# Down products with the upper halves one block ahead, later waits for expert vectors and padding, and logits placed among wide products

## The reference

```python
# 1. retention, per head, gamma = 1 - 2**(-5 - h)
state = gamma * state + k[t] v[t]^T
y[t] = scale * q[t] @ state
# 2. MLP, d_ff = 2048
h = x @ w_in
x = (maximum(h, 0) + alpha * minimum(h, 0)) @ w_out
# 3. top-1 mixture of 8 experts, d_ff = 1024
logits = (x / |x|) @ (emb / |emb|).T / tau
e = argmax(logits);  gate = softmax(logits)[e]
out = gate * (maximum(x @ w1[e], 0) @ w2[e])
```

## Time and profile before

| | us |
|---|---|
| median of 3 runs | 992.33 |
| lowest and highest | 988.33, 994.5 |
| the profiled execution | 989.66 |
| its span, first to last instruction | 987.8 |
| PE busy, PEld busy | 960.6 (97%), 794.4 (80%) |
| DVE, ACT, POOL busy | 579.2, 256.5, 241.3 |
| mean granted clock of TensorE | 0.993 of full |

### The profile page before, as it was taken

One profiled execution on the slowest core, in us unless ns is written; L12 is line 12 of the kernel. 1 busy time (PEld: TensorE's weight loads), 2 busy tenths in 40 slices (PEclk: granted clock), 3 DMA queues, 4 the chain that ended last, 5 costly groups with the idle time before them and its releaser, 6 DMA issues.

```text
span 987.8 us, 16560 instructions
## 1 busy us (share of the span) xinstructions
PE 960.6 (97%) x5448; PEld 794.4 (80%) x5449; DVE 579.2 (59%) x1079; ACT 256.5 (26%) x405; POOL 241.3 (24%) x192
## 2 busy tenths in 40 slices
PE   7999999999999999999999999999999999999994
PEld 6788778888887888878887888877888888888883
DVE  4655579637973698459864878664332742524541
ACT  4222121112111211122111212332333533423541
POOL 3443114241433133413441224210000110000000
PEclk9999999999999999999999999999999999999998
DMA  7431393023001400140011203446331361423310
GB/s 283 157 139 55 116 370 114 1 86 129 0 0 73 140 0 0 43 149 1 1 44 54 107 35 134 130 136 249 128 128 43 150 262 43 175 75 121 125 44 31
DMA packets 27122, 100.48 MB, mean 102 GB/s; under 512 B 4383, under 2 KB 4767, under 8 KB 22448
## 3 DMA queue, kind: packets, MB, share of 16 engines
q1 hardware_dynamic: 19136, 80.64, 22.8%
q0 software_dynamic: 4336, 12.61, 3.3%
q10 hardware_dynamic: 3600, 6.58, 2.4%
HBM read 87.19 MB, written 24.20 MB: 113 GB/s over the span
## 4 chain that ended last, share of the span: by engine, by line
PE 88%; DVE 4%; DMA 2%; SPq 1%; ACT 1%; issue 1%; POOL 1%; ACTq 0%; DVEq 0%; POOLq 0%
PE bank L684 25%; PE bank L675 25%; PE bank L759 14%; PE bank L785 14%; PE bank L571 2%; PE bank L770 2%; PE bank L617 2%; PE bank L587 1%; PE bank L660 1%; PE bank L604 1%; DMA en_all<-en_rows 1%; DVE scratch L898 1%; DVE scratch L903 1%; DMA en_all<-in_qk 1%; DVE activations_split L909 1%
## 5 line engine op out<-in xcount | busy, mean ns | idle before, releaser
L684 PE MATMUL bank<-weights_split,activations_split 128*128 128x512 f32 x1152 | 278.7, 391 | 4.9 <-DVE activations_split L909 4.7
L675 PE MATMUL bank<-activations_split,weights_split 128*128 128x512 f32 x1152 | 277.5, 391 | 0.4 <-issue 0.4
L684 PEld LDWEIGHTS bank<-weights_split,activations_split 128*128 128x128 f32 x1152 | 215.2, 188 | 54.6 <-DVE activations_split L909 7.8
L675 PEld LDWEIGHTS bank<-activations_split,weights_split 128*128 128x128 f32 x1152 | 215.1, 188 | 45.8 <-issue 1.5
L1478 POOL TENSOR_TENSOR activations_split<-scratch,activations_split 128x512 fp32r<-128x512 f32 x84 | 118.0, 1405 | 332.5 <-ACT activations_split L1266 325.1
L1266 ACT CAST activations_split<-scratch 128x512 fp32r<-128x512 f32 x96 | 59.8, 622 | 418.1 <-DVE scratch L903 418.1
L785 PE MATMUL bank<-weights_split,activations_split 128*128 (+1 forms) x648 | 154.9, 394 | 3.0 <-DVE activations_split L1130 2.2
L759 PE MATMUL bank<-weights_split,activations_split 128*128 (+1 forms) x648 | 156.8, 398 | 0.5 <-DVE activations_split L1107 0.5
L785 PEld LDWEIGHTS bank<-weights_split,activations_split 128*128 128x128 f32 x648 | 119.6, 188 | 27.5 <-issue 3.6
L759 PEld LDWEIGHTS bank<-weights_split,activations_split 128*128 128x128 f32 x648 | 121.3, 191 | 24.8 <-issue 0.7
L960 DVE SCALAR_TENSOR_TENSOR attention<-rows,en_all 128x512 f32<-128x512 f32 x140 | 135.0, 1006 | 0.0
(11 more groups left out here) (183 smaller groups left out, 678.4 us busy)
## 6 DMA issues: line engine op xcount, KB each, us to landing
attention<-in_w_exp SPq DMA_DIRECT2D x24, 1024.0 KB, 4.8
attention<-in_kv SPq DMA_DIRECT2D x43, 256.0 KB, 3.8
expert_rows<-in_pad_rows SPq DMA_DIRECT2D x8, 1028.0 KB, 18.3
en_all<-in_w_exp SPq DMA_DIRECT2D x8, 1024.0 KB, 7.1
rows<-in_w_mlp SPq DMA_DIRECT2D x14, 512.0 KB, 3.4
rows<-expert_rows ACTq DMA_DIRECT2D x25, 257.0 KB, 2.7
attention<-in_qk SPq DMA_DIRECT2D x12, 512.0 KB, 4.9
scratch<-in_qk SPq DMA_DIRECT2D x10, 512.0 KB, 3.7
```

The lines of the kernel that those rows point to most:

```text
L675: last = mm(H_ps[f % 2][:, :], win(a, kc, f), x[:, kc, :], start=(k == 0), stop=(k == 3 * KC - 1))
L684: last = mm(bank[j][:, :], x[f % 2][:, j * P:(j + 1) * P], wout(a, f), start=(f == 0 and n == 0), stop=(f == FB - 1 and n == 2))
```

## The change

In `down`, the twelve products of a block keep their operands but take another order: the two products with the upper half of the activations for group i come first, and the product with the lower half follows one group later. The block waits for `s_gh` at its start and for `s_gl` ahead of its fifth product. The order of the groups' last products is then 5th, 8th, 11th and 12th. `expert_down` does the same within each half of four feature blocks. In the first expert tile, the logits of group j are made behind the three products of feature block j of the second up half. DVE's wait for the expert vectors moves into `dots`, behind block 0's activations. ACT's wait for the padding moves behind `relu_half(2)` and `x_hi_part(3, 3)`, and the rows of tile 5 are loaded by SP instead of ACT.

```diff
--- before.py
+++ after.py
@@ -539,6 +539,7 @@
             sp.wait_ge(s_pad0, due(s_pad0, 16))
             sp.wait_ge(s_pads, due(s_pads, 16 * E))
             load_rows(sp, 1, 0)
+            load_rows(sp, 1, 1)
             with sp.Fori(2, E) as p:
                 e = sp.value_load(tab[0:1, bass.ds(T_PERM + p, 1)], min_val=0, max_val=E - 1)
                 for m in range(NCH):
@@ -677,13 +678,22 @@
                         k += 1
                 last.then_inc(s_h, 1)
 
+            def high_first(n):
+
+                order = []
+                for i in range(n):
+                    order += [(i, 0, "hi"), (i, 1, "hi")] + ([(i - 1, 0, "lo")] if i else [])
+                return order + [(n - 1, 0, "lo")]
+
             def down(c, f):
-                pe.wait_ge(s_gl, due(s_gl, FB * c + f + 1))
-                for j in range(B):
-                    for n, (a, x) in enumerate(((0, g_hi), (1, g_hi), (0, g_lo))):
-                        last = mm(bank[j][:, :], x[f % 2][:, j * P:(j + 1) * P], wout(a, f),
-                                  start=(f == 0 and n == 0), stop=(f == FB - 1 and n == 2))
-                    if f == FB - 1 and j < B - 1:
+                pe.wait_ge(s_gh, due(s_gh, FB * c + f + 1))
+                for n, (j, a, part_) in enumerate(high_first(B)):
+                    if n == 4:
+                        pe.wait_ge(s_gl, due(s_gl, FB * c + f + 1))
+                    x = g_hi if part_ == "hi" else g_lo
+                    last = mm(bank[j][:, :], x[f % 2][:, j * P:(j + 1) * P], wout(a, f),
+                              start=(f == 0 and a == 0 and part_ == "hi"), stop=(f == FB - 1 and part_ == "lo"))
+                    if f == FB - 1 and part_ == "lo" and j < B - 1:
                         last.then_inc(s_x2, 1)
                 last.then_inc(s_X, 1)
 
@@ -746,7 +756,7 @@
             def expert_of(t):
                 return pe.value_load(tab[0:1, bass.ds(T_EXP + t, 1)], min_val=0, max_val=E - 1)
 
-            def up(t, tt, half, e):
+            def up(t, tt, half, e, between=None):
                 slot = e % 2
                 if half == 0:
                     pe.wait_ge(s_el, due(s_el, t + 1))
@@ -760,7 +770,11 @@
                                   W[:, bass.ds(slot * HALF + w1_at(kc, a) + half * 512, 512)],
                                   start=(k == 0), stop=(k == 3 * KC - 1))
                         k += 1
+                    if between is not None and kc < KC - 1:
+                        between(kc)
                 last.then_inc(s_M1, 1)
+                if between is not None:
+                    between(KC - 1)
 
             def h_transpose(t):
                 for half in range(HF):
@@ -776,12 +790,14 @@
                 pe.wait_ge(s_lo[1], due(s_lo[1], HC * e))
                 pe.wait_ge(s_yd, due(s_yd, t))
                 k = 0
-                for fc in range(FC):
-                    if fc % 4 == 0:
-                        pe.wait_ge(s_hl, due(s_hl, 2 * t + fc // 4 + 1))
-                    if fc == FC // 2 and between is not None:
+                for half in range(HF):
+                    if half and between is not None:
                         between()
-                    for a, x in ((0, eh_hi), (1, eh_hi), (0, eh_lo)):
+                    pe.wait_ge(s_hh, due(s_hh, 2 * t + half + 1))
+                    for n, (i, a, part_) in enumerate(high_first(4)):
+                        if n == 4:
+                            pe.wait_ge(s_hl, due(s_hl, 2 * t + half + 1))
+                        x, fc = eh_hi if part_ == "hi" else eh_lo, 4 * half + i
                         last = mm(EY_ps[:, :], x[tt % 2][:, fc * P:(fc + 1) * P],
                                   W[:, bass.ds(slot * HALF + w2_at(fc, a), DM)],
                                   start=(k == 0), stop=(k == 3 * FC - 1))
@@ -803,9 +819,7 @@
             up(0, 0, 0, 0)
             for j in range(B):
                 last_transpose(j)
-            for j in range(B):
-                last_logits(j)
-            up(0, 0, 1, 0)
+            up(0, 0, 1, 0, between=last_logits)
             router_rank(NC - 1)
             mm(CNT_ps, ones, seen[:, :, B], start=True, stop=True).then_inc(s_cnt, 1)
             up(1, 1, 0, 0)
@@ -954,6 +968,8 @@
                 if first == 0:
                     dve.wait_ge(s_xeV, due(s_xeV, 2 * c + 2))
                     dve.wait_ge(s_xeA, due(s_xeA, 2 * c + 2))
+                    dve.wait_ge(s_en_all, due(s_en_all, 16))
+                    dve.wait_ge(s_en_last, due(s_en_last, 1))
                 for n in range(first, first + count):
                     j, e = n // E, n % E
                     dve.wait_ge(s_lg, due(s_lg, B * E * c + max(n - 1, 0)))
@@ -1089,8 +1105,6 @@
             ve.reciprocal(tau_sb[:, :], TAU_ps).then_inc(s_ent, 1)
 
             attention(1)
-            dve.wait_ge(s_en_all, due(s_en_all, 16))
-            dve.wait_ge(s_en_last, due(s_en_last, 1))
             def chunk(c):
                 mlp(c - 1, router_c=c - 2)
                 rows_out(c - 1)
@@ -1396,14 +1410,15 @@
             x_hi_part(2, 2)
             y_part(1, 0, 1)
             act.wait_ge(s_tab, due(s_tab, 1))
-            act.wait_ge(s_pads, due(s_pads, 16 * E))
             w1_part(next_expert(2), 1)
             relu_half(2)
             x_hi_part(3, 3)
+            act.wait_ge(s_pads, due(s_pads, 16 * E))
 
             def tile(i, tt, e):
                 t = 4 * i + tt
-                load_rows(act, i, tt + 3)
+                if not (isinstance(t, int) and t == 2):
+                    load_rows(act, i, tt + 3)
                 h_hi_part(t, tt)
                 e_next = next_expert(t + 1)
                 w1_part(e_next, t)
```

## The result

| | before | after |
|---|---|---|
| median | 991.83 us (4 runs, 988.33 to 994.5) | 980.59 us (4 runs, 979.11 to 981.26) |
| profiled execution | 989.66 | 980.66 |
| its span | 987.8 | 978.8 |

The ratio is 0.9896, with a 95% interval from 0.9871 to 0.992: faster by 1.0%. The forecast was 981.7 us, 1.1 us too high. The profiled executions are 9.0 us apart, where the sum said 10.6. So the total agrees better than its parts, and the parts are what is worth reading.

The account below looks back on a forecast made before the run. TensorE (PE), 88% of the chain, was taken as the bound, so time lay in its gaps and slow clock. Terms 2.3 + 5.5 + 0.75 - 0.4 + 1.0 + 0.75 + 0.7 = 10.6 us; 992.3 - 10.6 = 981.7 us, range 976 to 988.5.

Parts of the forecast that it names:

- The wait for the vectors: The 2.39 us gap before mlp(1)'s down products closes once DVE waits for the expert vectors later: 2.3 us gained.
- the ten gaps: Gaps before down products of each chunk's first and last hidden blocks close with upper halves first: 5.5 us gained.
- the POOL gaps: Two last-chunk gaps, 0.67 and 0.34 us, ended by POOL's low half, close: 0.75 us gained.
- kind (a): Gaps of 0.65 us before down products of a chunk's first and last hidden blocks, ended by DVE's low halves.
- The yardstick: A PEld gap is not lost whole, since the first load after it waits for nothing: 0.13 us off each gap.
- the second rival: In down blocks the fifth product still waits, its release costing 0.3 us: gain 8.1 us, 984.2 us; chance 10%.
- the third rival: Bank changes inside down blocks cost time: 480 more changes, up to 62 us, 1044 us; chance 3%.
- The end of a chunk: Banks complete later, so ACT's copies delay the start of attention in chunks 2 to 4: 0.4 us lost.
- The logits: Last chunk's logits among wide products: 1.0 us gained if the clock holds, despite a new 1.9 us rank-product stall.
- The first rival: The clock falls again around the last logits and rank products: about 3 us lost, 984.7 us; chance 22%.
- The padding: In the expert stage, ACT's later padding wait lets tile 2's relu finish before tile 3's transposes: 0.75 us gained.
- The last tile: Last expert tile's down products start on the upper half, shortening the 2.40 us gap: 0.7 us gained.

Follow-up runs that it names:

- vectors_alone: The kernel before with only DVE's wait for the expert vectors moved; 987.86 us, ratio 0.9977.
- upper_first_alone: The kernel before with only the new order and the two waits in the MLP's down products; 982.91 us, ratio 0.9918.
- padding_alone: The kernel before with only ACT's wait for the padding moved later and tile 5's rows loaded by SP; 987.9 us, ratio 0.9979.
- padding_undone: The changed kernel with ACT's wait for the padding and the row load put back as before; 980.27 us, ratio 0.9907.
- rank_later: The changed kernel with the rank and count products behind the next 12 wide products instead of ahead of them; 977.12 us, ratio 0.9873.
- gap_filled: The changed kernel with 8 extra wide products, whose result nobody reads, ahead of the rank products; 977.58 us, ratio 0.9879.
- table_later: rank_later with DVE's lower half of tile 0 and relu of tile 1 moved ahead of parts of the tile table; 975.64 us, ratio 0.9862.

## Why the prediction was right, and where it was not

**The wait for the vectors (2.3 us), the ten gaps (5.5), the POOL gaps (0.75): right.** Together 8.55 us were forecast and 8.77 measured. vectors_alone and upper_first_alone give 1.73 and 7.27. The first is less than the 2.3 because without the new gate 0.65 us of kind (a) stays in that gap, just as the forecast split it; their sum, 9.0, is 0.2 above the 8.77 of both together. The yardstick of 0.13 us off each gap held: 10.2 us of gaps (7.8 + 1.4 + 1.0) went, and 8.77 were gained, 0.11 less for each of the 13. The lower half was in time for the fifth product in every block of the MLPs, so the second rival is excluded. The 0.3 us release at the expert's down products was no price of a wait in the middle of a block. It is there again where PE stands idle: 0.3 us from ACT's upper half (962.21) to the last tile's down loads (962.51). For the third rival the new order was counted wrong: 7 changes of bank in a block and not 8, so 384 more changes and not 480, and 28 ns each instead of 22 would have decided. Measured, a change costs nothing.

**The end of a chunk (-0.4 us): wrong, it was 0.** from_state starts 1.44 us after the last down loads end (214.03 - 212.59), 1.45 before (218.59 - 217.14). I had moved the end of ACT's copies by the 0.45 us that bank 2 is later. But the second copy reads bank 3, which is complete with the twelfth product in either order; before, it had waited for it, and that wait was inside the 1.26 us (ACT is idle for nearly all of the tenth from 217.5 to 217.6). Now the first copy starts later, the second follows at once, and both take 1.07 us. They end at 213.89, 0.14 us before from_state.

**The logits (+1.0 us): wrong in sign, -1.7 in the profile.** The step that failed is "if the clock holds". The loads, the 1.9 us stall and the end of the rank products came as worked out. The first rival, with a chance of 22%, had the mechanism and put the cost of the fall at about 3 us; measured, 1.0 + 1.7 = 2.7. It is also the one of the forecast's signs of being wrong that came: a lower clock, 0.50 from 635 to 641 us, where the stall was to leave it at 1.00. The argument against it was the idle stretch at 970 to 971 with a clock of 1.00. That one row was taken for a rule. upper_first_alone shows the same gap at the same place, 2.40 us, followed by the lower level. Whether a stall of about 2 us costs the clock differs from one profile to the next, so one that got through says little. In all six profiles that have the new stall of 1.86 us, the block behind it was slow (3.95 to 4.81 us). In the five with the old arrangement it was slow in four and not in the fifth. So the edit didn't prevent the fall, and added a stall of 1.86 us. That the fall also became more regular rests on one profile of the five.

**The padding (+0.75 us): right for the edit alone, not in the changed kernel.** padding_alone saves 0.79 us in its profile and 1.8 in the median. In the changed kernel the edit is worth nothing that could be measured, and that the table shows 0.79 beside a forecast of 0.75 is luck: in padding_undone that gap is closed without it. The step that failed is "so the engine behind the padding isn't helped, and PE keeps its 1.0 us": it took PE to come sooner by 1.0 us while the padding moved by 0.2, and PE came 2.01 us later while the padding's issue moved by 1.58. A saving at a gap depends on when both sides arrive, and another edit had moved one of them.

**The last tile (+0.7 us): right,** 0.71 (2.40 - 1.69).

**The base.** The median of 3 runs, 992.33, was high: 46 later runs of the same kernel have medians near 989.6. By those, the gain is 9.1 us, and the sum of 10.6 was 1.5 too large. In the profile the logits are 2.7 us short of the sum, the MLPs 0.6 and the start 0.6 above it. Counted from 989.7, the sum would have given 979.1, 1.5 us too low; a base 2.7 us too high turned that into 1.1 us too high. That 981.7 lies so near to 980.59 is luck: two errors of opposite sign.

**The chances.** Faster by over 1% was given 0.50, and the ratio 0.9896 is 1.04%: it sits on the boundary, as the forecast said it would. The interval reaches to both sides of one per cent, and against the 46 later runs of the kernel before the gain is 0.9%.

## What to carry to other kernels

When an operand arrives in two halves, put the wait for each half ahead of the first product that reads it and order the products so that the late half comes last; here that was worth 7 us of 617 at no cost in pace. Before moving thin work into a stretch of wide work, ask what wide work was covering the wait behind it: filling a stall of 1.9 us, even with useless products, was worth 3 us because it kept the clock; moving wide products ahead of it that had stood behind it was worth as much without added work. And take gains at two gaps as additive only if neither edit moves the other gap's two sides against each other.

## What the runs showed of the hardware that was not expected

**The clock falls behind short gaps, not every time.** Four places lost it: the vectors' gap (2.23 us, next 12 loads 4.04 us instead of 2.59), the rank products' stall (1.86 us, 4.81), the padding's gap (2.04 us, 24 loads 6.93 instead of 5.30) and the last tile's (2.40 us, 6.94 instead of 5.33). Each fall costs 1.5 to 2.9 us, and each place has another profile in which the clock held or fell less. The length of the gap isn't all: the stall of 1.86 us, with thin products before and behind it, lost the clock in all six profiles that have it, while the last tile's gap lost it in one of five at 2.4 us and in none of nine at 1.7 us.

**This is where the spread of the times seems to come from.** The kernel before ranges over 7 us in the first set, from 987.4 (mean granted clock 0.995) to 994.37 (0.989). Over its 46 runs the time goes with the mean clock: on average 991.2 us at 0.991 (7 runs), 989.5 at 0.993 (22), 987.9 at 0.995 (3). An estimate from these numbers fits: a mean clock lower by 0.006 is some 12 us of the span at half clock, in which about 6 us of work are lost, and the two ends lie 7 us apart. The three kernels whose stall at the logits is filled or moved, rank_later, gap_filled and table_later, have a mean clock of 0.996 or 0.997 in every run and a range of 0.35 to 0.72 us. The link is by the mean clock of each run; only the profiled executions show the place of the falls.

**What costs nothing.** 11 changes of PSUM bank in a block of 12 products, and one more wait in the middle of each of the 96 blocks that is met in time: the chain shows 2.72 us a block with and without them.
